# Second product of MLP 1 by Strassen's seven products, and spatial weights prepared in MLP 2

## The chip, the cores and the metric

One core of a Trainium2 chip runs the whole program. The metric is the device time of one execution in microseconds; lower is better. Everything is float32 on the host. TensorE works on fp32r copies: each operand is split in a high part and a low part (value minus high part), and a product is three matmuls, high x high, low x high, high x low.

## The reference

```python
# attention, 4 batches x 8 heads x 576 x 64, with rotary q and k; then, per batch of 576 x 512:
xn = (x - mu) / np.sqrt(var + 1e-06) * g_ln          # MLP 1
x = x + np.maximum(xn @ w_ch1, 0.0) @ w_ch2          # 512 -> 2048 -> 512
h = gelu(x @ w_in)                                   # MLP 2, 512 -> 1024
u, v = (h[..., :512], h[..., 512:])
v_n = (v - mu) / np.sqrt(var + 1e-06) * g_ln
v_s = np.einsum('ts,bsd->btd', w_sg, v_n) + b_sg[None, :, None]
x = x + (u * v_s) @ w_out
```

## The kernel before

The program has three stages: attention over 16 pairs of heads, written as software-pipelined rounds; MLP 1; MLP 2. Each engine has its own instruction stream, in an order written out by hand, and waits on semaphores. Data of all stages stays in SBUF.

MLP 1 works in five blocks of rows. Block 0 and blocks 2 to 4 hold the first 512 rows of one batch each (`block_tiles` = 4 tiles of 128 rows); block 1, the tails block, holds the last 64 rows of the four batches in 2 tiles. All 2048 hidden features are 16 tiles (NF). In a block TensorE alternates `hidden(n, f)` (L1624, matmul at L1637: 12 matmuls of 512 columns, 256 in the tails block, one PSUM bank of two) with `project(n, f - 1)` (L1642, matmul at L1652: 4 row tiles x 3 matmuls of 512 columns into the four banks of `acc_ps`, which gather over all 16 f). Between them ScalarE's relu writes the high part of `hid` (L946) and DVE the low part (L1268). At the end of a block DVE adds the four banks to Y (L1288).

The next block's input is made beside this: DVE's statistics at f = 4, GpSimd's `inverse_std` (L759, the power -0.5), DVE's `normalise` at f = 8 (L1175); then TensorE transposes xhat in four groups (`transpose_x`, L1576), two before the last-but-one `project` and two before the last, into the two banks of `xT_ps`; ScalarE (L933) and DVE (L1183) read each bank out as high and low part of xT. Block 0's x is transposed during attention.

Weights of MLP 1: SP loads slices of W1 and W2 for one f at a time into two raw slots (L644, L645); in block 0 ScalarE writes the high parts (L938, L939) and DVE the low parts (L1242, L1244), two f ahead; GpSimd did the first two f during the last rounds of attention. They stay in SBUF for all blocks. `hidden(0, 0)` stands in the last round of attention; behind the rounds come `transpose_o_tails` (L1661, the attention output of the tails, 16 transposes), DVE's merging of them (L1259), `hidden(0, 1)`, `project(0, 0)` and so on.

In the last block w_in and w_out are loaded and split between the steps (L961, L966, L1297, L1302); at f = 10 to 14 TensorE also transposes the spatial weights w_sg in five groups (`transpose_spatial`, L1700) into `xT_ps`, ScalarE (L975) and DVE (L1309) split them into wsT; and at the end Y of batch 0 is transposed (L1710, L1717) and split (L994, L1318).

MLP 2 goes batch by batch: `v_tiles` (L1737, 12 matmuls of 512 columns per row tile), `u_chunks` (L1757), the transposes of the next batch, `spatial` (L1775), the next batch's `v_tiles`, `outputs` (L1789). Each v tile goes through gelu on ScalarE (L1011) and, in DVE's queue, `v_stats` (L1335, L1337, L1339), GpSimd's power (L812) and `v_normal` (L1344, L1350, L1352); DVE takes the statistics of tile t ahead of the normalising of tile t - 1.

## Time and profile before

| | |
|---|---|
| median of 3 runs | 941.87 us (940.79 to 942.12) |
| the profiled execution's own time | 940.78 us |
| its span | 939.0 us |
| granted TensorE clock | 1.0 of full speed (2.4 GHz) over the span |
| attention | up to about 313 us |
| MLP 1 | about 313 to 720 us |
| MLP 2 | about 720 us to the end |

The span is what the profiler's records cover; the remaining 1.8 us of the execution lie around it. Engines are named PE (TensorE matmul), PEld (its weight loads), DVE, ACT (ScalarE), POOL (GpSimd), SPq (the queue that issues DMAs). Matmuls overlap, so that the duration of one is longer than the distance to the next.

### The profile page before, as it was taken

How to read it: one execution, taken by the hardware profiler on the slowest of the kernel's cores; microseconds unless marked ns; L12 is line 12 of the kernel's file. 1: busy time of each engine (PE TensorE's matmuls, PEld its weight loads, DVE VectorE, ACT ScalarE, POOL GpSimd, SP SyncE). 2: the span in 40 equal slices, each digit the busy share in tenths (PEclk: the TensorE clock that was granted, in tenths of full speed). 3: DMA queues.
4: the chain of work that ended last, by engine and by line, in shares of the span. 5: the costliest groups of instructions: out<-in, count | busy, mean ns of one | idle time of the engine just before them, and what ended most of it. 6: DMA issues, size and time to landing. Idle time of an engine off the chain costs nothing.

```text
span 939.0 us, 15729 instructions
## 1 busy us (share of the span) xinstructions
PE 914.4 (97%) x5577; PEld 820.3 (87%) x5577; DVE 510.9 (54%) x903; ACT 400.0 (43%) x857; POOL 269.2 (29%) x249
## 2 busy tenths in 40 slices
PE   4899999999999999999999999999999999999998
PEld 3899999999989888898888888888888999989897
DVE  5899999999998644232222322132235663663623
ACT  4899999999988332211111111121123221302110
POOL 4989989989863000000000000000000110010100
PEclk9999999999999999999999999999999999999999
DMA  6243243233222332100000000003100001010011
GB/s 177 65 103 93 66 102 91 64 102 92 67 56 71 105 100 90 68 1 1 1 1 0 1 0 0 0 1 114 45 1 1 1 1 45 2 45 13 1 45 57
DMA packets 44966, 44.24 MB, mean 47 GB/s; under 512 B 14128, under 2 KB 34864, under 8 KB 44784
## 3 DMA queue, kind: packets, MB, share of 16 engines
q1 hardware_dynamic: 44480, 43.21, 16.5%
q8 instruction: 35, 0.57, 0.2%
q10 hardware_dynamic: 432, 0.30, 0.1%
q14 instruction: 19, 0.16, 0.1%
HBM read 28.81 MB, written 4.72 MB: 36 GB/s over the span
## 4 chain that ended last, share of the span: by engine, by line
PE 91%; DVE 4%; issue 1%; POOL 1%; ACT 1%; DMA 0%; SPq 0%; POOLq 0%; ACTq 0%; DVEq 0%
PE hid_ps L1637 21%; PE acc_ps L1652 21%; PE ring_ps L1545 8%; PE wide_ps L1775 6%; PE scores_ps L1481 6%; PE wide_ps L1757 5%; PE ring_ps L1492 5%; PE bank_ps L1789 5%; PE bank_ps L1737 5%; PE scores_ps L1474 2%; PE ring_ps L1428 2%; DVE nmax L1105 1%; PE ring_ps L1558 1%; PE ring_ps L1503 1%; DVE prob_lo L1114 1%
## 5 line engine op out<-in xcount | busy, mean ns | idle before, releaser
L1652 PE MATMUL acc_ps<-W2s,hid 128*128 128x512 f32 x864 | 210.6, 391 | 0.1
L1637 PE MATMUL hid_ps<-xT,W1s 128*128 128x512 f32 (+1 forms) x960 | 210.4, 369 | 0.3 <-DVE xT L1183 0.3
L1637 PEld LDWEIGHTS hid_ps<-xT,W1s 128*128 128x128 f32 x960 | 168.6, 188 | 31.9 <-issue 0.7
L1652 PEld LDWEIGHTS acc_ps<-W2s,hid 128*128 128x128 f32 x864 | 160.5, 188 | 33.1 <-DVE hid L1268 0.8
L1268 DVE SCALAR_TENSOR_TENSOR hid<-hid_ps,hid 128x512 fp32r<-128x512 f32 (+1 forms) x80 | 51.0, 638 | 253.1 <-ACT hid L946 253.0
L946 ACT ACTIVATE hid<-hid_ps 128x512 fp32r<-128x512 f32 (+1 forms) x80 | 44.4, 555 | 304.3 <-PE hid_ps L1637 304.3
L1105 DVE TENSOR_REDUCE nmax<-scores_ps 128x1 f32<-128x576 f32 x144 | 106.8, 752 | 14.1 <-PE scores_ps L1481 10.3
L812 POOL TENSOR_TENSOR rstd<-ve,power 128x1 f32<-128x1 f32 x18 | 14.6, 814 | 306.1 <-DVE ve L1339 306.1
L855 ACT ACTIVATE E<-scores_ps,nmax 128x576 f32<-128x576 f32 x128 | 95.7, 749 | 11.5 <-DVE nmax L1105 10.8
L1114 DVE TENSOR_TENSOR prob_lo<-ring_ps,prob_hi 128x512 fp32r<-128x512 f32 x144 | 95.4, 681 | 2.1 <-ACT prob_hi L869 1.7
L869 ACT ACTIVATE prob_hi<-ring_ps 128x512 fp32r<-128x512 f32 x144 | 85.6, 613 | 2.3 <-PE ring_ps L1492 0.9
L1481 PE MATMUL scores_ps<-stack 128*128 128x288 f32 x256 | 80.1, 328 | 0.9 <-ACT E L855 0.9
L1492 PE MATMUL ring_ps<-ident,E 128*128 128x128 f32 x512 | 76.7, 276 | 1.5 <-DVE prob_lo L1114 1.4
L759 POOL TENSOR_TENSOR rstd<-ve,power 128x4 f32<-128x4 f32 (+1 forms) x5 | 4.8, 954 | 251.7 <-DVE ve L1168 251.7
L1545 PE MATMUL ring_ps<-prob_hi,v_split 128*128 128x288 f32 x256 | 76.2, 316 | 0.2 <-DVE prob_lo L1114 0.2
L1481 PE MATMUL scores_ps<-swapped_k,stack 128*128 128x288 f32 x256 | 72.2, 297 | 0.0
L1545 PE MATMUL ring_ps<-prob_lo,v_split 128*128 128x288 f32 x256 | 70.8, 295 | 0.0
L1492 PEld LDWEIGHTS ring_ps<-ident,E 128*128 128x128 f32 x512 | 58.7, 140 | 3.6 <-issue 1.8
L1775 PE MATMUL wide_ps<-wsT,v_hat 128*128 128x288 f32 x448 | 60.3, 295 | 0.0
L1775 PEld LDWEIGHTS wide_ps<-wsT,v_hat 128*128 128x128 f32 x448 | 59.6, 188 | 0.0
L1757 PEld LDWEIGHTS wide_ps<-yT,winS 128*128 128x128 f32 x384 | 51.3, 188 | 0.3
L1757 PE MATMUL wide_ps<-yT,winS 128*128 128x288 f32 x384 | 51.5, 294 | 0.0
(142 smaller groups left out, 1441.6 us busy)
## 6 DMA issues: line engine op xcount, KB each, us to landing
swapped_k<-stack SPq DMA_DIRECT2D x64, 144.0 KB, 2.4
w_raw<-in_w SPq DMA_DIRECT2D x32, 256.0 KB, 3.0
qk_raw<-in_k SPq DMA_DIRECT2D x16, 256.0 KB, 2.7
v_raw<-in_v SPq DMA_DIRECT2D x16, 256.0 KB, 2.8
qk_raw<-in_q SPq DMA_DIRECT2D x15, 256.0 KB, 2.8
out<-out_sb SPq DMA_DIRECT2D x14, 256.0 KB, 2.2
w_raw<-in_win SPq DMA_DIRECT2D x4, 512.0 KB, 4.2
rotary<-rotary_table SPq DMA_DIRECT2D x2, 576.0 KB, 4.3
```

What stands on the lines that cost most here:

```text
L855: nc.scalar.activation(dst, src, ACT.Exp, bias=nmax[:, s:s + 1], accum_out=rowsum[:, p.odd, s:s + 1]).then_inc(expd, 1)
L869: nc.scalar.activation(dst, src, ACT.Copy).then_inc(prob_hi_s, 1)
L1105: nc.vector.tensor_reduce(nmax[:, s:s + 1], scored(p, s), axis=AX.X if s == NT else AX.XY, op=ALU.max, negate=True).then_inc(maxed, 1)
L1114: read_out(nc.vector.tensor_tensor(dst, src, hi.bitcast(f32), ALU.subtract), job, h)
L1268: nc.vector.scalar_tensor_tensor(out=hid[:, f % 2, 1, 0:cols], in0=hid_ps[:, f % 2, 0:cols], scalar=0.0, in1=hid[:, f % 2, 0, 0:cols].bitc ...
L1481: mm = nc.tensor.matmul(ps[:, half, 0:HALF], queries, keys, start=(m == 0), stop=(m == 1))
L1492: mm = nc.tensor.transpose(bank(f"G{t}", h)[:, P * c:P * c + P], E[:, t, at + P * c:at + P * c + P], ident[:, :])
L1545: mm = nc.tensor.matmul(bank(job, h)[:, 0:HALF], values, moving, start=(c == 0 and n == 0), stop=(c == NT and n == 1))
L1637: mm = nc.tensor.matmul(hid_ps[:, f % 2, 0:cols], W1s[:, slot1(f), w, c, :], xT[:, x, c, 0:cols], start=first, stop=(c == DC - 1 and x == 1))
L1652: mm = nc.tensor.matmul(acc_ps[:, t, :], hid[:, f % 2, x, P * t:P * t + P], W2s[:, slot2(f), w, :], start=(f == 0 and x == 0 and w == 0), ...
L1757: mm = nc.tensor.matmul(wide_ps[j % 2][:, half, 0:HALF], winS[:, c, w, P * j:P * j + P], yT[:, a, c, HALF * half:HALF * (half + 1)], start ...
L1775: mm = nc.tensor.matmul(wide_ps[j % 2][:, half, 0:HALF], v_hat[:, a, c, P * j:P * j + P], wsT[:, w, c, HALF * half:HALF * (half + 1)], sta ...
```

## The change

The second product of MLP 1 goes by pairs of hidden tiles (g, eight of them) and pairs of row tiles. The 2x2 blocks are: hidden tiles 2g and 2g + 1 against even and odd row tiles on the left, W2's two row tiles against the two halves of its 512 columns on the right. Seven products of (128 rows x 128) by (128 x 256), by the variant of Strassen's method with 4 + 4 sums ahead, gather in seven PSUM banks `seven_ps` over all g. The left factors (`lefts`) come from ScalarE's relu and high parts and DVE's four sums and five low parts; the right factors (`rights`), made anew for every pair in every block, from GpSimd's four sums of W2 and four low parts, ScalarE's five high parts and one low part on DVE. `lefts`, `rights`, `w2_sums`, `hid`, `hid_sums` have one buffer each. At the end of a block eight `fold` steps on DVE, two copies on ScalarE and four additions on GpSimd bring the seven banks into Y. W2 is no longer split as a whole; it is kept raw, loaded for two f at a time.

With seven banks taken, one bank (`fc1_ps`) is left for `hidden` and for the four groups of x transposes, which now stand one by one between products. Half of `transpose_o_tails` stands behind `hidden(0, 1)`. The spatial weights are transposed and split inside `v_tiles(0)` and use the banks of `wide_ps`, which `u_chunks(0)` needs next. The blocks, which were in part a loop, are written out. The core of the diff, with the outer indentation taken off (in the order SP, GpSimd, ScalarE, DVE, TensorE):

```diff
-hid = sbuf(m1, "hid", [P, 2, 2, NT * P], f32r)
+hid = sbuf(m1, "hid", [P, 2, NT * P])
+hid_sums = sbuf(m1, "hid_sums", [P, 4, 2 * P])
 W1s = sbuf(m1, "W1s", [P, NF, 2, DC, P], f32r)
-W2s = sbuf(m1, "W2s", [P, NF, 2, DM], f32r)
+w2_rest = sbuf(m1, "w2_rest", [P, NF - 2, DM])
+lefts = sbuf(m1, "lefts", [P, SEVEN, 2, 2 * P], f32r)
+folds = sbuf(m1, "folds", [P, 2, 4 * P])
+rights = sbuf(m1, "rights", [P, SEVEN, 2, 2 * P], f32r)
+w2_sums = sbuf(m1, "w2_sums", [P, 4, 2 * P])
...
-acc_ps = psum(m1_ps, "acc_ps", [P, NT, 512])
-hid_ps = psum(m1_ps, "hid_ps", [P, 2, 512])
-xT_ps = psum(m1_ps, "xT_ps", [P, 2, 512])
+seven_ps = {n: psum(m1_ps, f"seven_ps{n}", [P, 512]) for n in range(3, SEVEN)}
+fc1_ps = psum(m1_ps, "fc1_ps", [P, 512])
+seven_ps.update({n: psum(m1_ps, f"seven_ps{n}", [P, 512]) for n in range(3)})
...
+SPATIAL = ((), (0, 1), (2,), (3,), (4,))
...
+def y_bank(b, c):
+    return bank_ps[0 if b == 0 else c]
...
+LEFT_PARTS = (1, 2, 3, 3, 4, 5, 5)
+FOLDS = 8
+FREE_FOLDS = (3, 2, 4, 5, 6, 7, 8)
...
-        sp.wait_ge(w_lo, max(2 * (f - 1), 4))
+        sp.wait_ge(w_lo, f - 1)
         load_weights(f)
-    sp.wait_ge(w_lo, 2 * NF)
-    for c in range(2):
-        sp.dma_start(pass_raw[c], win_v[:, c, :]).then_inc(raw_in[c], 16)
-    sp.wait_ge(fc2, (NBLK - 1) * NF + SG1)
-    sp.dma_start(wsg_raw[:, 0:NT, :], wsg[0:NT * P, :].rearrange("(p t) s -> p t s", t=NT)).then_inc(wsg_in, 16)
...
+        if f == 2:
+            wait_filled(sp, pair(PAIRS - 1), ("PV0", 0), ("PV1", 0), ("PV0", 1), ("PV1", 1))
+        if f % 2 == 0:
+            sp.dma_start(w2_rest[:, f - 2:f, :], w2_v[:, f:f + 2, :]).then_inc(w2_in[f // 2 - 1], 16)
+    def wait_rights(count):
+        sp.wait_ge(right_lo, 4 * count)
+        sp.wait_ge(right_lo_sums, count)
+    sp.wait_ge(w_lo, NF)
+    sp.dma_start(pass_raw[0], win_v[:, 0, :]).then_inc(raw_in[0], 16)
+    wait_rights((NBLK - 1) * NG + 1)
+    sp.dma_start(pass_raw[1], win_v[:, 1, :]).then_inc(raw_in[1], 16)
     for c in range(2, DC):
         sp.wait_ge(mw_lo, c - 1)
         sp.dma_start(pass_raw[c % 2], win_v[:, c, :]).then_inc(raw_in[c % 2], 16)
     for c in range(0, DC, 2):
         sp.wait_ge(mw_lo, DC - 1 + c // 2)
...
+    wait_rights((NBLK - 1) * NG + 5)
...
+    def weight_sums(n, g):
+        at = n * NG + g
+        if at == 0:
+            pool.wait_ge(scores, PAIRS * NQK)
+            pool.wait_ge(w_in[1], 32)
+        if n == 0 and g > 0:
+            pool.wait_ge(w2_in[g - 1], 16)
+        if at > 0:
+            pool.wait_ge(right_lo_sums, at)
+            pool.wait_ge(right_lo, 4 * at)
+        sums = [w2_sums[:, m, :] for m in range(4)]
+        w11, w12, w21, w22 = [w2_block(g, f, half) for f in range(2) for half in range(2)]
+        nc.gpsimd.tensor_tensor(sums[T3], w22, w12, ALU.subtract).then_inc(w2_summed, 1)
+        nc.gpsimd.tensor_tensor(sums[T1], w12, w11, ALU.subtract).then_inc(w2_summed, 1)
+        pool.wait_ge(w2_summed, 4 * at + 2)
+        nc.gpsimd.tensor_tensor(sums[T2], w22, sums[T1], ALU.subtract).then_inc(w2_summed, 1)
+        pool.wait_ge(w2_summed, 4 * at + 3)
+        nc.gpsimd.tensor_tensor(sums[T4], sums[T2], w21, ALU.subtract).then_inc(w2_summed, 1)
+    def right_low(n, g, k):
+        pool.wait_ge(right_hi, 5 * (n * NG + g) + {0: 1, 1: 2, 2: 3, 6: 5}[k])
+        src = {0: w2_block(g, 0, 0), 1: w2_sums[:, T3, :], 2: w2_block(g, 1, 0), 6: w2_block(g, 1, 1)}[k]
+        nc.gpsimd.tensor_tensor(rights[:, k, 1, :], src, rights[:, k, 0, :].bitcast(f32), ALU.subtract).then_inc(right_lo, 1)
+    def add_to_y(n, odd, half, m, wait):
+        pool.wait_ge(folded, FOLDS * n + wait)
+        y = y_block(n, odd, half)
+        nc.gpsimd.tensor_tensor(y, y, fold_view(n, folds[:, m, :]), ALU.add).then_inc(y1_done, 1)
+    weight_sums(0, 0)
+    for k in (0, 1, 2, 6):
+        right_low(0, 0, k)
+    for n in range(NBLK):
+        for g in range(NG):
+            ahead = after(n, g)
+            if ahead[0] < NBLK:
+                weight_sums(*ahead)
+                for k in range(3):
+                    right_low(*ahead, k)
+            if g == NG - 1:
+                add_to_y(n, 1, 1, 0, 2)
+            if ahead[0] < NBLK:
+                right_low(*ahead, 6)
+            if g == 3 and not is_last(n):
+                inverse_std(n + 1)
+        pool.wait_ge(y1_done, 4 * n + 1)
+        add_to_y(n, 1, 1, 1, 6)
+        add_to_y(n, 1, 0, 0, 7)
+        add_to_y(n, 0, 1, 1, 8)
...
-    def weights_high(f):
-        act.wait_ge(w_in[f % 2], 32 * (f // 2 + 1))
+    def w1_high(f):
+        act.wait_ge(w_in[f % 2], 16 * (f // 2 + 2))
         nc.scalar.activation(W1s[:, slot1(f), 0, :, :], w1_raw[:, f % 2, :, :], ACT.Copy).then_inc(w_hi, 1)
-        nc.scalar.activation(W2s[:, slot2(f), 0, :], w2_raw[:, f % 2, :], ACT.Copy).then_inc(w_hi, 1)
...
+    def relu(n, g, f):
+        at = n * NG + g
         cols = P * block_tiles(n)
+        act.wait_ge(fc1, 2 * at + f + 1)
+        if at > 0:
+            if f == 0:
+                act.wait_ge(hid_summed, 4 * (at - 1) + 3)
+            else:
+                act.wait_ge(left_lo, 5 * (at - 1) + 3)
+        nc.scalar.activation(hid[:, f, 0:cols], fc1_ps[:, 0:cols], ACT.Relu).then_inc(hid_relu, 1)
...
+    def left_high(n, g, part):
+        at = n * NG + g
+        wait_product(n, g, (0, 1, 3, 4, 6)[part])
...
+        nc.scalar.activation(dst, src, ACT.Copy).then_inc(left_hi, 1)
...
+    def right_high(n, g, part):
+        at = n * NG + g
+        wait_product(n, g, (0, 1, 2, 5, 6)[part])
...
+        if part == 1:
+            act.wait_ge(w2_summed, 4 * at + 1)
+        if part == 3:
+            act.wait_ge(w2_summed, 4 * at + 4)
+            dst, src = rights[:, 3:6, 0, :], w2_sums[:, T4:T2 + 1, :]
+        else:
+            dst = rights[:, (0, 1, 2, 0, 6)[part], 0, :]
+            src = {0: w2_block(g, 0, 0), 1: w2_sums[:, T3, :], 2: w2_block(g, 1, 0), 4: w2_block(g, 1, 1)}[part]
+        nc.scalar.activation(dst, src, ACT.Copy).then_inc(right_hi, 1)
...
+    def copy_fold(n, m):
+        k = (0, 4)[m]
+        act.wait_ge(fc2, SEVEN * (n * NG + NG - 1) + k + 1)
+        if n > 0:
+            act.wait_ge(y1_done, 4 * n)
+        nc.scalar.activation(folds[:, m, 0:2 * P * block_pairs(n)], seven(n, k), ACT.Copy).then_inc(fold_copied, 1)
...
+    def factors(n, g):
+        first, last = n > 0 and g == 0, g == NG - 1
+        if first:
+            copy_fold(n - 1, 0)
+        if n == 0 and g == 0:
+            w1_high(2)
+            for part in range(5):
+                right_high(0, 0, part)
+        relu(n, g, 0)
+        if n == 0 and 0 < g and 2 * g + 2 < NF:
+            w1_high(2 * g + 2)
+        left_high(n, g, 0)
+        right_high_beside(n, g, 0)
+        if last:
+            relu(n, g, 1)
+        left_high(n, g, 1)
+        right_high_beside(n, g, 1)
+        if last:
+            next_high(n, 0)
+        right_high_beside(n, g, 2)
+        if first:
+            copy_fold(n - 1, 1)
+        if not last:
+            relu(n, g, 1)
+        if n == 0 and 2 * g + 3 < NF:
+            w1_high(2 * g + 3)
+        left_high(n, g, 2)
+        if last:
+            next_high(n, 1)
+        left_high(n, g, 3)
+        right_high_beside(n, g, 3)
+        if last:
+            next_high(n, 2)
+        left_high(n, g, 4)
+        right_high_beside(n, g, 4)
+        if last:
+            next_high(n, 3)
+            next_high(n, 4)
...
+    def spatial_high(c):
+        if c == 0:
+            act.wait_ge(y1_done, 4 * NBLK)
+        act.wait_ge(wsT_ps, c + 1)
...
+    def hid_sum(n, g, m):
+        at = n * NG + g
+        if m == S3:
+            if at > 0:
+                dve.wait_ge(left_lo, 5 * at)
+            dve.wait_ge(hid_relu, 2 * at + 1)
+            a, b, op = hid_rows(n, 0, 0), hid_rows(n, 1, 0), ALU.subtract
+        elif m == S1:
+            dve.wait_ge(hid_relu, 2 * at + 2)
+            a, b, op = hid_rows(n, 1, 0), hid_rows(n, 1, 1), ALU.add
+        elif m == S2:
+            dve.wait_ge(hid_summed, 4 * at + 2)
+            a, b, op = sum_rows(n, S1), hid_rows(n, 0, 0), ALU.subtract
+        else:
+            dve.wait_ge(hid_summed, 4 * at + 3)
+            a, b, op = hid_rows(n, 0, 1), sum_rows(n, S2), ALU.subtract
+        nc.vector.tensor_tensor(sum_rows(n, m), a, b, op).then_inc(hid_summed, 1)
+    def left_low(n, g, part):
+        dve.wait_ge(left_hi, 5 * (n * NG + g) + part + 1)
...
+        nc.vector.tensor_tensor(dst, src, high.bitcast(f32), ALU.subtract).then_inc(left_lo, 1)
...
+    def fold(n, step):
+        k = (0, 1, 0, 2, 3, 5, 5, 6)[step]
+        dve.wait_ge(fc2, SEVEN * (n * NG + NG - 1) + k + 1)
+        if step in (0, 1, 5):
+            dve.wait_ge(fold_copied, 2 * n + 1 + step // 5)
...
+    def factors(n, g):
+        first, last = n > 0 and g == 0, g == NG - 1
+        if first:
+            for step in range(4):
+                fold(n - 1, step)
+        if n == 0 and g == 0:
+            w1_low(2)
+            merge_tails((0, 1))
+        hid_sum(n, g, S3)
+        left_low(n, g, 0)
+        if n == 0 and 0 < g and 2 * g + 2 < NF:
+            w1_low(2 * g + 2)
+        if not last:
+            left_low(n, g, 1)
+        if first:
+            fold(n - 1, 4)
+        if n == 0 and g == 0:
+            w1_low(3)
+            merge_tails((2, 3))
+            right_low_sums(0, 0)
+        hid_sum(n, g, S1)
+        hid_sum(n, g, S2)
+        hid_sum(n, g, S4)
+        if last:
+            left_low(n, g, 1)
+            next_low(n, 0)
+        left_low(n, g, 2)
+        if n == 0 and 0 < g and 2 * g + 3 < NF:
+            w1_low(2 * g + 3)
+        if last:
+            next_low(n, 1)
+        left_low(n, g, 3)
+        if n > 0 or g > 0:
+            right_low_sums(n, g)
+        if first:
+            fold(n - 1, 5)
+            fold(n - 1, 6)
+        if last:
+            next_low(n, 2)
+        left_low(n, g, 4)
+        if first:
+            fold(n - 1, 7)
+        if last:
+            next_low(n, 3)
+            next_low(n, 4)
...
             if t > 0:
                 v_normal(jobs_tv(b) + t - 1, b, t - 1)
+            if b == 0 and t < count:
+                for c in SPATIAL[t]:
+                    spatial_low(c)
...
+            elif c == 0:
+                pe.wait_ge(hid_relu, n * NF)
             else:
-                if isinstance(n, int) and n == 1 and c < 2:
-                    wait_bank_done((1, 2)[c])
-                head_wait(pe, xT_lo, n, DC, c - 1)
+                pe.wait_ge(xT_lo, n * DC + c)
...
-    def project(n, f):
-        pe.wait_ge(hid_lo, n * NF + f + 1)
-        if f == 0:
-            head_wait(pe, y1_done, n, 1, 0)
-            if isinstance(n, int) and n == 0:
-                pe.wait_ge(tails_merged, B)
-                pe.wait_ge(w_lo, 4)
-        for t in range(block_tiles(n)):
+    def product(n, g, k):
+        at = n * NG + g
+        pe.wait_ge(left_lo, 5 * at + LEFT_PARTS[k])
+        if 3 <= k < 6:
+            pe.wait_ge(right_lo_sums, at + 1)
+        else:
+            pe.wait_ge(right_lo, 4 * at + min(k + 1, 4))
+        if g == 0 and n > 0:
+            pe.wait_ge(folded, FOLDS * (n - 1) + FREE_FOLDS[k])
+        elif g == 0 and k < 3:
+            wait_bank_done(k)
+        elif g == 0:
+            pe.wait_ge(tails_merged, B)
+        for a in range(block_pairs(n)):
             for x, w in ((0, 0), (1, 0), (0, 1)):
-                mm = nc.tensor.matmul(acc_ps[:, t, :], hid[:, f % 2, x, P * t:P * t + P], W2s[:, slot2(f), w, :],
-                                      start=(f == 0 and x == 0 and w == 0), stop=(f == NF - 1 and w == 1))
+                mm = nc.tensor.matmul(seven_ps[k][:, 2 * P * a:2 * P * (a + 1)], lefts[:, k, x, P * a:P * (a + 1)],
+                                      rights[:, k, w, :], start=(g == 0 and a == 0 and x == 0 and w == 0),
+                                      stop=(g == NG - 1 and a == block_pairs(n) - 1 and w == 1))
         mm.then_inc(fc2, 1)
...
+    def products(n, g):
+        steps = [("fc1", 0), 0, 1, 2, ("fc1", 1), 3, 4, 5, 6]
+        if g == NG - 2:
+            steps = [("fc1", 0), 0, ("fc1", 1), 1, ("x", 0), 2, 3, ("x", 1), 4, 5, ("x", 2), 6]
+        elif is_last(n) and g == NG - 1:
+            steps = [0, ("x", 3), 1, 2, ("tails", 0), 3, 4, 5, 6]
+        elif g == NG - 1:
+            steps = [0, ("x", 3), 1, 2, ("fc1", 0), 3, 4, ("fc1", 1), 5, 6]
+        m, h = after(n, g)
...
     rounds(pe, body, (-2, 1))
-    transpose_o_tails()
-    def mlp1_block(n):
...
-            if f == NF - 1 and not is_last(n):
-                transpose_x(n + 1, range(2))
...
-            project(n, f - 1)
-            if is_last(n) and SG2 < f <= SG2 + NTT:
-                transpose_spatial(f - SG2 - 1)
-        if not is_last(n):
-            transpose_x(n + 1, range(2, DC))
-        else:
...
+    transpose_o_tails((0, 1))
+    hidden(0, 1)
+    transpose_o_tails((2, 3))
...
     def transpose_spatial(c):
         if c == 0:
             pe.wait_ge(wsg_in, 32)
-        else:
-            pe.wait_ge(wsT_lo, c)
+            pe.wait_ge(folded, FOLDS * NBLK)
+        if c >= 2:
+            pe.wait_ge(wsT_lo, c - 1)
         rows = P if c < NT else TAIL
-        dst = xT_ps[:, :, :].rearrange("p a n -> p (a n)")
+        dst = wide_ps[c % 2][:, :, :].rearrange("p a n -> p (a n)")
...
+            if b == 0:
+                for c in SPATIAL[t]:
+                    transpose_spatial(c)
...
             elif b > 0:
                 pe.wait_ge(sg_bias, DC * b - 1 + j)
-            elif j == 0:
-                pe.wait_ge(y1_done, NBLK)
+            else:
+                pe.wait_ge(wsT_lo, NTT - j)
```

## Rows read from the trace of the kernel before

**Rows 1.** The page: busy time by engine, and the chain that ended last.

```profile
PE 914.4 (97%) x5577; PEld 820.3 (87%) x5577; DVE 510.9 (54%) x903; ACT 400.0 (43%) x857; POOL 269.2 (29%) x249
...
PE 91%; DVE 4%; issue 1%; POOL 1%; ACT 1%; DMA 0%; SPq 0%; POOLq 0%; ACTq 0%; DVEq 0%
```

**Rows 2.** Groups by shape, PE: count | busy us, mean ns | idle before.

```profile
L1652 PE MATMUL acc_ps<-W2s,hid 128*128 128x512 f32 x864 | 210.6, 391 | 0.1
...
L1637 PE MATMUL hid_ps<-xT,W1s 128*128 128x256 f32 x192 | 25.4, 283 | 0.0
```

**Rows 3.** PE's timeline (start us, us) in block 3 and in the tails block.

```profile
634.26 2.88 PE L1637 MATMUL hid_ps<-xT,W1s 128*128 128x512 f32 x12
636.98 2.88 PE L1652 MATMUL acc_ps<-W2s,hid 128*128 128x512 f32 x12
...
404.98 1.59 PE L1637 MATMUL hid_ps<-xT,W1s 128*128 128x256 f32 x12
406.41 1.55 PE L1652 MATMUL acc_ps<-W2s,hid 128*128 128x512 f32 x6
407.80 1.59 PE L1637 MATMUL hid_ps<-xT,W1s 128*128 128x256 f32 x12
```

**Rows 4.** Groups by shape, POOL, with two inputs in SBUF.

```profile
L712 POOL TENSOR_TENSOR cross<-qk_raw,rotary 128x288 f32<-128x288 f32 x60 | 47.5, 818 | 0.0
...
L768 POOL TENSOR_TENSOR W1s<-w_raw,W1s 128x512 fp32r<-128x512 f32 x2 | 2.6, 1302 | 0.2
```

**Rows 5.** Timeline 12 to 14.2 us, DVE and POOL; and one line's min/median/max.

```profile
12.19 0.41 DVE L1062 TENSOR_TENSOR qk_split<-rot,qk_split 128x256 fp32r<-128x256 f32 x1
...
12.78 1.40 POOL L697 TENSOR_TENSOR rot<-qk_raw,rotary 128x576 f32<-128x576 f32 x1 [11.79 <-DVE qk_split L1062]
12.84 1.61 DVE L1062 TENSOR_TENSOR qk_split<-rot,qk_split 128x256 fp32r<-128x256 f32 x1
...
14.13 0.98 POOL L712 TENSOR_TENSOR cross<-qk_raw,rotary 128x288 f32<-128x288 f32 x1
...
L712 POOL TENSOR_TENSOR cross<-qk_raw,rotary x4: 792/806/982, 14.1 to 18.0; 128x288 f32<-128x288 f32 x4
```

**Rows 6.** PE's timeline at the end of block 0: x transposes for the tails block.

```profile
394.04 0.60 PE L1576 MATMUL xT_ps<-ident,xhat 128*128 128x128 f32 x4
394.39 3.00 PE L1652 MATMUL acc_ps<-W2s,hid 128*128 128x512 f32 x12
397.24 0.60 PE L1576 MATMUL xT_ps<-ident,xhat 128*128 128x128 f32 x4
```

**Rows 7.** Groups by shape, ACT and DVE.

```profile
L933 ACT ACTIVATE xT<-xT_ps,g1c 128x512 fp32r<-128x512 f32 x12 | 7.6, 686 | 5.7 <-PE xT_ps L1576 5.6
...
L1183 DVE SCALAR_TENSOR_TENSOR xT<-xT_ps,g1c,xT 128x512 fp32r<-128x512 f32 x12 | 8.4, 746 | 5.5 <-ACT xT L933 5.5
...
L1242 DVE TENSOR_TENSOR W1s<-w_raw,W1s 128x512 fp32r<-128x512 f32 x14 | 9.7, 691 | 4.2 <-ACT W2s L939 4.2
...
L1309 DVE TENSOR_TENSOR wsT<-xT_ps,wsT 128x576 fp32r<-128x576 f32 x4 | 3.0, 758 | 8.4 <-ACT wsT L975 8.4
```

**Rows 8.** Timeline at the start of MLP 1, all engines.

```profile
310.44 0.58 SPq L644 DMA_DIRECT2D w_raw<-in_w  x1
...
314.13 0.63 ACT L938 ACTIVATE W1s<-w_raw 128x512 fp32r<-128x512 f32 x1 [0.82 <-DMA w_raw<-in_w]
...
314.62 3.02 PE L1637 MATMUL hid_ps<-xT,W1s 128*128 128x512 f32 x12
```

**Rows 9.** Timelines: spatial transposes in block 4; start of MLP 2.

```profile
683.22 0.89 PE L1700 MATMUL xT_ps<-ident,wsg_raw 128*128 128x128 f32 x5
...
733.81 12.88 PE L1757 MATMUL wide_ps<-yT,winS 128*128 128x288 f32 x96
...
729.20 0.69 DVE L1335 BATCH_NORM_STATS2 stats<-v_act 128x6 f32<-128x512 f32 x1
...
731.25 0.69 DVE L1352 TENSOR_TENSOR v_hat<-v_act,v_hat 128x512 fp32r<-128x512 f32 x1
```

425 lines of the change are left out of this document (257 added, 168 removed).

## The prediction

> **What bounds the kernel now.** I read the page's busy shares and the chain that ended last first: TensorE is busy 97% of the span and carries 91% of the chain [rows 1]. Then the groups by shape: the second product is 864 matmuls of 512 columns [rows 2]. Then TensorE's timeline for the pitch, which a busy sum hides since matmuls overlap: in a block of four tiles 12 matmuls start every 2.72 us, 227 ns each; in the tails block 12 of 256 columns start every 1.43 us (119 ns), 6 of 512 every 1.39 us [rows 3]. Nothing waits there. So TensorE's time is the kernel's, column or wait alike. Last I read what one DVE, ScalarE or GpSimd instruction takes, as the change gives these three work in every step.
>
> **Part 1, matmuls.** Per pair of hidden tiles a full block goes from 24 matmuls of 512 columns (5.44 us) to 7x2x3 = 42 of 256. At 119 ns [rows 3] that is 5.01 us: 0.43 saved, 32 times, 13.9 us. In the tails block 12 of 512 (2.78) become 21 of 256 (2.50): 8x0.28 = 2.2. Together **-16.1 us**. (Columns fall by 1/8, but each matmul carries some 13 ns besides them, and their number rises from 864 to 1512.)
>
> **Part 2, GpSimd, and its port with DVE.** Each pair of hidden tiles gives GpSimd eight instructions of 256 columns (four sums of W2, four low parts), in every block anew. Its rows give 818 ns for 288 columns and 1302 for 512 [rows 4], so about 0.75 for 256, and back to back they follow some 50 ns closer (14.13 against an end at 14.18 [rows 5]): 0.70. Two of the sums wait for the one before, 0.15 each: 5.9 us per pair. A full block's pair takes TensorE 5.44+5.01 = 10.45 us, so there it is hidden. The tails block's takes 2.86+2.50 = 5.4: **GpSimd becomes the bound**, since w2_sums and rights have one buffer and weight_sums waits for all low parts of the pair before.
> DVE's new instructions (four sums, five low parts of the left, one of the right) have both inputs in SBUF. The trace has such a one against GpSimd: the subtraction of 256 columns takes 0.41 us alone, but 1.61 where it starts 0.06 us after a GpSimd instruction that ends at 14.18, and the next GpSimd instruction takes 0.98 where its like take 0.81 [rows 5]. They don't run together. So DVE takes from GpSimd 0.17 for 256 columns. A tails pair has 2176 such columns: 1.4 us in proportion, 2.3 at the 1.08 ns per column that 0.41 for 256 and 0.69 for 512 [rows 7] make; I take 1.9. Period 5.9+1.9 = 7.8.
> From the Trainium skill, SBUF — State Buffer, section "Who interferes with whom": the port pair is an exclusive lock held for the whole instruction, where a DVE instruction has two SBUF inputs and GpSimd reads SBUF. By that to the letter the whole durations add up, and the period would be about 9 us, the total 8 us more than below; the row shows GpSimd losing less, and I keep 7.8.
> The tails block, from its predecessor's last product: fc1 and products of the first pair 5.5 us, but GpSimd has first three additions into Y of 512 columns (1.3 each [rows 4], the first after DVE's sixth fold at about 2.2) till 6.0, then four sums and a low part, 3.7 and 0.7 for DVE's holds, so that product 0 of the second pair can start at 10.4 and the pair ends at 15.4. Four periods of 7.8 to the sixth; 1.0 for inverse_std in GpSimd's queue; then two pairs with x transposes. There each step must pass transposes 0.60, ScalarE 0.69, DVE 0.75 and handshakes 0.1, 2.15 us to the next step [rows 6, 7], before the single bank fc1_ps is free, while TensorE has only 1.2 us of other work (0.35 transposes, 0.13 for the switch, two products of 0.36): with the 512-column fc1 of the next block 20.5 us for the two pairs. 15.4+31.2+1.0+20.5 = 68.1 against 47.4 of pure TensorE work (14x1.43, 2x2.72, 8x2.50, transposes 1.9): **+20.7**. Bounds: +5 (GpSimd hidden, only the x chain waits) and +35 (period 9.3).
>
> **Part 3, x transposes between full blocks.** Before, eight transposes stood together in two banks, and four cost 0.35, with 0.13 for the switch to matmuls and back (2.85 to the next start instead of 2.72) [rows 6]. Now four at a time share one bank with fc1. The same chain of 2.15 is met by 1.92 of cover (0.35+0.13+2x0.72): 0.2 short per step. DVE's queue has three sums and a low part ahead of the first low part of x (+0.3), the right's low part of 768 columns ahead of the third (+0.3), and fc1 waits for relu twice (+0.3); two more switches (+0.2): 1.7, and 1.0 for GpSimd in DVE's way. Two such boundaries 5.4; into the tails block 2.9; y's transposes at the end 2.8: **+11.1**. Bounds +4 and +16. At a full block's start the folds (8x0.69 on DVE [rows 7], beside 3584 columns of its own, 3.9, in the 10.4 us of a pair) and additions are met by nearly a whole pair of slack: **+1.0** for both, bounds 0 and 4.
>
> **Part 4, start.** ScalarE's order puts W1's third slice and five high parts of the right ahead of relu(0,0). The slice is issued at 310.44 and was cast at 314.13 (then also behind W2's) [rows 8]; without W2 I take 313.4. 0.5+1.8 us of copies, relu 0.6: hidden(0,1), which before started at 314.62 behind all tail transposes, now waits till 316.4 where TensorE is ready at 313.8. Product 2 then waits 0.7 for DVE (W1 low, merges, right low, three sums). Less the wait of 0.5 that goes: **+2.8**, bounds 0 and 5. SP's queue keeps its order there; W2's 0.5 MB loads are a pair ahead of use. W2's splits (14 each on ScalarE and DVE) go; they lay beside TensorE and give nothing back.
>
> **Part 5, spatial weights.** 25 transposes move from the last block into v_tiles(0); TensorE's cost is the same. u_chunks(0) now waits for the fifth low part, behind gelu, statistics and the normalising of a tile in DVE's queue: gelu with its handshake 0.8, statistics to low part 729.20 to 731.94 = 2.74 [rows 9], wsT 0.76 [rows 7], handshakes 0.1, less the 0.89 of the transposes beside it [rows 9]: **+3.5**, bounds 2.5 and 5. Spatial products of batch 0 have the u products, 12.9 us [rows 9], before them. SP's loads of w_in, w_out and w_s now wait for rights or low parts of the last block, each at least a pair of 10.4 us ahead of its use, and its queue has nothing else then: 0; if one came late, every later load behind it would too. ScalarE: 12 instructions with 4608 columns, 6.2 us per full pair at the 0.69 for 512 of [rows 7], in 10.4: hidden. Unrolled blocks: only instruction fetch, 0.
>
> **Sum:** -16.1+20.7+11.1+1.0+2.8+3.5 = +23.0. The profiled execution has 940.78 (span 939.0), 1.1 below the median of 941.87: 963.8, on the median's scale 964.9. Some of these waits will overlap with one another, so I say **960**.
>
> **Rivals.**
> A, the cover holds: GpSimd and DVE run far enough ahead, transposes hide; only start and end cost. 941.9-16.1+6.3 = 932. For it: they idle most of this stage today. Against: single buffers keep them from running ahead, and 5.9 > 5.4. Chance 0.12. It decides if GpSimd's 256 columns take 0.6 or less and DVE is not in its way.
> B, the port costs nothing, as today in MLP 1, where GpSimd idles: period 5.9 (4x1.9 less, and about 2 more where the block starts and ends), no 1.0 at each of four boundaries: 963.8-13.6 = 950. Chance 0.18. Against it: rows 5.
> C, the lock also fills the full blocks: GpSimd 5.9, DVE's 3584 two-input columns 3.9 and in block 0 its W1 parts, 10 and more, with waits for each other's ends: 1 us over on 32 pairs, 995. Chance 0.09. Decides where a full pair's period passes 10.45.
> D, Strassen saves nothing: if 256 columns cost 132 ns, as their busy sum over count says (25.4/192) [rows 2], 42 take 5.55, more than 5.44; 1512x0.013 = 20 us more than my case, 980. The timeline (12 in 1.43) speaks against. Chance 0.03.
> E, waits just use up the saving: 942. Chance 0.05.
> My own case, 950 to 975: 0.53.
>
> **Numbers.** The range leaves out A and C (0.21) and holds the bounds of the big terms in part: 938 to 985. What this kernel's measurement can tell from no change is about 0.2%, 1.9 us. Faster 0.13 (A and a little of B's lower side), same 0.05, slower 0.82.
>
> **What would show it.** (1) Product rows of 256 columns pitched 0.119. (2) In the tails block a period near 7.8, GpSimd busy nearly throughout, TensorE waiting for the right's low part. (3) GpSimd rows of 256 columns longer than 0.75 on average and DVE rows of 256 with two SBUF inputs up to 1.1 long. (4) TensorE waits of 0.2 to 1 before each x transpose group. (5) One wait of 3 to 4 us before the first u product; one of 2 to 3 before hidden(0,1). I am wrong if GpSimd's rows stay at 0.74 and the tails block keeps TensorE's pace, or if full pairs exceed 10.45 in the middle of a block.

## The result, and the profile after

The changed kernel takes 984.4 us (median of 4 runs, 982.35 to 985.15) against 942.0 for the kernel before on the same chip: ratio 1.045, 95% interval 1.043 to 1.047. The forecast was 960, slower; the direction is right and 984.4 lies in the range of 938 to 985, at its edge. The rise is 42 us where the working gave 23, so most of this section and the next is about the other 20. The profiled execution, the longest of the four, has a span of 983.4. Below, fc1 is the first product of MLP 1 (`hidden`, twelve matmuls), and x transposes are the four groups that prepare the next block's input.

The page of the kernel after, busy time and chain, against [rows 1]:

```profile
PE 928.7 (94%) x6225; PEld 857.4 (87%) x6225; DVE 755.3 (77%) x1231; ACT 566.4 (58%) x1253; POOL 570.0 (58%) x585
...
PE 79%; DVE 12%; ACT 3%; issue 2%; POOL 2%; DMA 1%; SPq 0%; ACTq 0%; DVEq 0%; POOLq 0%
```

DVE now carries 12% of the chain, GpSimd only 2%. That is the first sign against the prediction, which had named GpSimd. The next lines are windows of MLP 1, cut where the first fc1 of a block starts; they hold block 0, the tails block, block 2 and block 3. Their columns are: window, us, then busy us and count of TensorE, its weight loads, DVE, ScalarE, GpSimd; granted clock; DMA share and GB/s.

```profile
310.99:407.21 96.22, 88.80 (x535) 78.68 (x533) 77.13 (x115) 53.21 (x116) 57.59 (x67) 0.96 0.28 83
...
407.21:481.14 73.93, 57.26 (x391) 54.39 (x389) 63.78 (x107) 38.24 (x102) 57.86 (x71) 0.86 0.00 1
481.14:570.91 89.77, 88.06 (x533) 78.20 (x533) 66.26 (x107) 48.39 (x102) 58.14 (x69) 0.98 0.00 1
570.91:659.81 88.90, 87.19 (x544) 78.18 (x544) 72.58 (x107) 48.69 (x102) 61.46 (x70) 1.00 0.00 1
```

Block 3 takes 88.9, as a full block did before (88.86 between the same places): what the products save there is given back at the block's end, no more and no less. The tails block takes 73.9, with TensorE busy 57 of them and DVE 64; TensorE's work in that window, some 390 matmuls at the pitch of 0.12, is about 46 (an estimate). Now TensorE's timeline, against [rows 3, 6, 8]: the start of MLP 1, a full pair, and the tails block from its fourth pair.

```profile
318.13 4.42 PE L1986 MATMUL fc_ps<-xT,W1s 128*128 128x512 f32 x12 [2.93 <-ACT hid L1066]
...
329.98 0.98 PE L2007 MATMUL seven_ps<-rights,lefts 128*128 128x256 f32 x6 [2.23 <-DVE lefts L1529]
330.80 4.51 PE L1986 MATMUL fc_ps<-xT,W1s 128*128 128x512 f32 x12
335.15 3.03 PE L2007 MATMUL seven_ps<-rights,lefts 128*128 128x256 f32 x24
338.02 2.91 PE L1986 MATMUL fc_ps<-xT,W1s 128*128 128x512 f32 x12
...
440.01 2.40 PE L1986 MATMUL fc_ps<-xT,W1s 128*128 128x256 f32 x12 [3.31 <-ACT hid L1066]
...
457.45 2.70 PE L1986 MATMUL fc_ps<-xT,W1s 128*128 128x256 f32 x12 [4.59 <-ACT hid L1066]
```

24 matmuls of 256 columns, 335.15 to 338.02, are pitched 0.12, as forecast, and a full pair lasts 10.51 (335.15 to 345.66). But twelve fc1 matmuls of 512 columns last 4.42 and 4.51 behind a wait and 2.91 elsewhere. The granted clock (the last column but two) is below 1.00 there, so the engine ran in part at 1.2 GHz:

```profile
315.00:320.00 5.00, 2.07 (x7) 1.51 (x6) 3.88 (x9) 3.79 (x9) 3.25 (x4) 0.78 0.83 267
330.00:335.00 5.00, 5.00 (x18) 4.10 (x19) 3.52 (x6) 2.10 (x6) 3.02 (x4) 0.66 0.10 30
```

And TensorE waits in the tails block for ScalarE's relu. The relu stands behind a left part in ScalarE's queue, and these parts wait for DVE's sums of hid, 15.6 us in 422 to 474:

```profile
L1088 ACT ACTIVATE lefts<-hid_sums 128x128 fp32r<-128x128 f32 x12 | 3.7, 310 | 15.8 <-DVE hid_sums L1517 15.6 <-PE seven_ps L2007 0.2
```

The groups by shape of DVE, then of GpSimd, against [rows 4, 5, 7]:

```profile
L1517 DVE TENSOR_TENSOR hid_sums<-hid 128x256 f32<-128x256 f32 x64 | 47.4, 741 | 45.7 <-ACT hid L1066 45.5
...
L1529 DVE TENSOR_TENSOR lefts<-hid,lefts 128x256 fp32r<-128x256 f32 x40 | 32.8, 819 | 0.1
...
L1554 DVE TENSOR_TENSOR Y<-seven_ps,Y 128x512 f32<-128x512 f32 x20 | 13.2, 680 | 0.1
```

```profile
L898 POOL TENSOR_TENSOR rights<-w_rest,rights 128x256 fp32r<-128x256 f32 x105 | 97.7, 933 | 74.9 <-ACT rights L1107 74.9
```

DVE's 256 columns with two inputs in SBUF take 0.74 and 0.82 in these groups (0.62 to 0.64 in the other three) where 0.41 is the time alone, while a 512-column one with an input in PSUM stays at 0.68. In MLP 2 the forecast wait of 3.5 stands as 3.60, and the 96 u products behind it take 14.28 instead of 12.9:

```profile
775.70 14.28 PE L2130 MATMUL wide_ps<-yT,winS 128*128 128x288 f32 x96 [3.60 <-DVE wsT L1650]
```

### The profile page after: what moved, and what is told of

Its sections match the earlier page's. It is cut to its first block, busy times and chain, and to the rows that moved or that the text cites. A ratio compares the mean times of both kernels' runs of the same rounds, so it can differ in the third digit from the quotient of the medians.

```text
span 983.4 us, 18631 instructions
## 1 busy us (share of the span) xinstructions
PE 928.7 (94%) x6225; PEld 857.4 (87%) x6225; DVE 755.3 (77%) x1231; ACT 566.4 (58%) x1253; POOL 570.0 (58%) x585
## 4 chain that ended last, share of the span: by engine, by line
PE 79%; DVE 12%; ACT 3%; issue 2%; POOL 2%; DMA 1%; SPq 0%; ACTq 0%; DVEq 0%; POOLq 0%
PE fc_ps L1986 18%; PE seven_ps L2007 13%; PE ring_ps L1893 7%; PE scores_ps L1829 6%; PE wide_ps L2151 6%; PE wide_ps L2130 5%; PE ring_ps L1840 5%; PE bank_ps L2165 5%; PE bank_ps L2107 4%; DVE hid_sums L1517 3%; PE scores_ps L1822 2%; PE ring_ps L1776 2%; DVE lefts L1529 1%; DVE xT L1421 1%; ACT rights L1107 1%
## 5 line engine op out<-in xcount | busy, mean ns | idle before, releaser
L1986 PE MATMUL fc_ps<-xT,W1s 128*128 128x512 f32 (+1 forms) x960 | 221.5, 382 | 15.3 <-ACT hid L1066 14.6
L1986 PEld LDWEIGHTS fc_ps<-xT,W1s 128*128 128x128 f32 x960 | 170.3, 197 | 46.6 <-ACT hid L1066 13.9
L2007 PE MATMUL seven_ps<-rights,lefts 128*128 128x256 f32 x1512 | 204.2, 288 | 2.8 <-DVE lefts L1529 2.2
L2007 PEld LDWEIGHTS seven_ps<-rights,lefts 128*128 128x128 f32 x1512 | 196.6, 195 | 8.9 <-DVE lefts L1529 2.9
L898 POOL TENSOR_TENSOR rights<-w_rest,rights 128x256 fp32r<-128x256 f32 x105 | 97.7, 933 | 74.9 <-ACT rights L1107 74.9
L1088 ACT ACTIVATE lefts<-hid_sums 128x256 fp32r<-128x256 f32 (+2 forms) x120 | 54.8, 457 | 78.8 <-DVE hid_sums L1517 71.1
L1517 DVE TENSOR_TENSOR hid_sums<-hid 128x256 f32<-128x256 f32 (+1 forms) x80 | 56.6, 707 | 50.9 <-ACT hid L1066 50.4
L1066 ACT ACTIVATE hid<-fc_ps 128x512 f32<-128x512 f32 (+1 forms) x80 | 44.0, 550 | 82.4 <-PE fc_ps L1986 82.3
L1529 DVE TENSOR_TENSOR lefts<-hid_sums,lefts 128x256 fp32r<-128x256 f32 (+2 forms) x120 | 86.0, 717 | 2.2 <-ACT lefts L1088 2.2
L1529 DVE TENSOR_TENSOR lefts<-hid,lefts 128x256 fp32r<-128x256 f32 (+1 forms) x80 | 62.8, 785 | 0.1
```

The source lines that it names most:

```text
L898: nc.gpsimd.tensor_tensor(rights[:, k, 1, :], src, rights[:, k, 0, :].bitcast(f32), ALU.subtract).then_inc(right_lo, 1)
L1517: nc.vector.tensor_tensor(sum_rows(n, m), a, b, op).then_inc(hid_summed, 1)
L1529: nc.vector.tensor_tensor(dst, src, high.bitcast(f32), ALU.subtract).then_inc(left_lo, 1)
L1986: mm = nc.tensor.matmul(fc1_ps[:, 0:cols], W1s[:, slot1(f), w, c, :], xT[:, x, c, 0:cols], start=first, stop=(c == DC - 1 and x == 1))
L2007: mm = nc.tensor.matmul(seven_ps[k][:, 2 * P * a:2 * P * (a + 1)], lefts[:, k, x, P * a:P * (a + 1)], rights[:, k, w, :], start=(g == 0 an ...
```

## The experiments

e1 to e4 and e8 are single executions. The changed kernel's own four lie 2.8 us apart, so these five are read from their blocks first and from their totals second.

**Whose work fills the tails block (e1, e2).** Theory 1: DVE and GpSimd block each other there, DVE's bursts add waits, and the lost clock adds time. Two kernels leave one side's work out, all but 8 columns of each instruction, without a change in order or waits.

```diff
# e1: GpSimd's sums and low parts, e2: DVE's sums and low parts of the tails block
+cols = slice(0, 8 if n == 1 else 2 * P)
-nc.gpsimd.tensor_tensor(rights[:, k, 1, :], src, ...)
+nc.gpsimd.tensor_tensor(rights[:, k, 1, cols], src[:, cols], ...)
```

> Leaves out: in the tails block GpSimd's eight instructions of a pair (four sums of W2, four low parts) work on 8 of their 256 columns; order and semaphores stay. The tails block takes 74.5 us (without the fc1 of its successor above a tails fc1) where pure TensorE work is 47.4. Theory 1 (the shared port lengthens DVE's instructions, DVE's bursts stop the hidden sums, and each TensorE idle stretch costs clock as well): DVE's rows of 128 and 256 columns in that block fall to 0.29 and 0.42, the block to 60 to 66, the kernel to 970 to 976. Rival, GpSimd's amount of work bounds the period: the block to 50 to 55, the kernel to 960 to 965. Rival, ScalarE and the handshakes bound it: under 4 us less, 980 or more.

> Leaves out: in the tails block DVE's four sums of hid, five low parts of the left and the low part of the right work on 8 columns of each row group; GpSimd's work, statistics, normalising and folds stay. Theory 1: GpSimd's 256-column rows in that block fall from 0.80 to 0.90 towards 0.74; the waits behind the statistics, the normalising and the folds stay (2 to 4 us each, three of them), as does the low clock behind them; the block falls from 74.5 to 62 to 68, the kernel to 971 to 978. Rival, GpSimd bounds it by itself: the block falls by under 4. Rival, DVE's small work bounds it: the block to 50 to 55, the kernel to 960 to 965.

Without GpSimd's columns: 968.97 us, the tails block 58.1. Its window, and DVE's groups in its middle (421.4 to 458):

```profile
407.91:465.97 58.06, 50.57 (x391) 48.76 (x389) 42.68 (x107) 37.36 (x102) 22.67 (x69) 0.95 0.01 1
```

```profile
L1519 DVE TENSOR_TENSOR hid_sums<-hid 128x128 f32<-128x128 f32 x13 | 3.9, 302 | 7.8 <-ACT hid L1068 7.6
...
L1531 DVE TENSOR_TENSOR lefts<-hid,lefts 128x256 fp32r<-128x256 f32 x6 | 2.5, 419 | 0.0
L1395 DVE BATCH_NORM_STATS2 stats<-Y 128x6 f32<-128x512 f32 x4 | 2.5, 673 | 0.0
...
L1415 DVE TENSOR_SCALAR xhat<-Y,mv,rstd 128x512 f32<-128x512 f32 x4 | 1.9, 546 | 0.9 <-POOL rstd L837 0.9
```

The same groups of the changed kernel (422 to 474):

```profile
L1517 DVE TENSOR_TENSOR hid_sums<-hid 128x128 f32<-128x128 f32 x13 | 7.8, 600 | 4.5 <-ACT hid L1066 4.3
L1529 DVE TENSOR_TENSOR lefts<-hid,lefts 128x256 fp32r<-128x256 f32 x7 | 5.6, 802 | 0.0
...
L1413 DVE TENSOR_SCALAR xhat<-Y,mv,rstd 128x512 f32<-128x512 f32 x4 | 3.5, 944 | 0.6 <-POOL rstd L837 0.6
L1393 DVE BATCH_NORM_STATS2 stats<-Y 128x6 f32<-128x512 f32 x4 | 2.5, 674 | 0.0
```

DVE did the same instructions in 42.7 instead of 63.8 us: 21 us of DVE's "busy" time in that block was waiting for GpSimd. Without DVE's columns the kernel takes 973.56, the block 64.6, and GpSimd's low parts go from 828 to 747 ns. Its timeline shows how GpSimd holds DVE:

```profile
434.70 0.74 POOL L898 TENSOR_TENSOR rights<-w_sums,rights 128x256 fp32r<-128x256 f32 x1
434.87 0.60 DVE L1518 TENSOR_TENSOR hid_sums<-hid_sums,hid 128x8 f32<-128x8 f32 x1
435.40 0.75 POOL L898 TENSOR_TENSOR rights<-w_rest,rights 128x256 fp32r<-128x256 f32 x1
435.50 0.67 DVE L1518 TENSOR_TENSOR hid_sums<-hid,hid_sums 128x8 f32<-128x8 f32 x1
436.10 0.16 DVE L1534 TENSOR_TENSOR lefts<-hid,lefts 128x16 fp32r<-128x16 f32 x1
```

A DVE instruction of 8 columns that needs 0.16 lasts 0.60 and 0.67, until GpSimd's ends. Four pairs in the middle of the tails block, in the changed kernel, in e1 and in e2 (columns as above):

```profile
422.08:457.45 35.37, 27.04 (x180) 26.04 (x180) 31.35 (x55) 17.60 (x48) 29.19 (x37) 0.86 0.00 1
421.38:446.85 25.47, 23.59 (x180) 23.19 (x181) 18.75 (x55) 16.95 (x48) 9.02 (x34) 0.93 0.01 2
420.86:450.39 29.53, 24.03 (x180) 22.18 (x181) 20.43 (x55) 17.18 (x48) 26.66 (x37) 1.00 0.01 1
```

The block without GpSimd's columns came out 2 us below what theory 1 expected, the other within it; the rival "ScalarE and handshakes" is out, since the block falls by 16; "GpSimd by itself bounds it" is out, since taking DVE's columns away gives 9.4; so is "DVE's small work bounds it", which wanted 50 to 55. Neither side alone accounts for the block.

**Bursts or sums (e3).** The same work with DVE's statistics one tile per pair, and the normalising in two halves.

```diff
-elif g == 2:
-    for t in range(block_tiles(n + 1)):
-        tile_statistics(n + 1, t)
+elif g < 4:
+    t = g - 4 + block_tiles(n + 1)
+    if t >= 0:
+        tile_statistics(n + 1, t)
...
-elif g == 4:
-    normalise(n + 1)
+elif g < 6:
+    normalise(n + 1, range(half * (g - 4), half * (g - 3)))
```

> The same work in another order: in every block DVE takes the statistics of one tile per pair of hidden tiles (pairs 0 to 3) and normalises half of the tiles behind pair 4 and half behind pair 5, instead of all at once behind pair 2 and pair 4. Theory 1: the waits of 3.3 and 4.6 us before fc1 in the tails block shrink to under 1 us each, and the 2.4 to 2.5 us that the fc1 behind them takes goes back to 1.6; the block loses 6 to 9 us, the kernel comes to 975 to 979. Rival, the block is bound by GpSimd's eight instructions: they fill the gap, the block loses under 2. Other stages stay within 1 us.

978.4 us, within the expected numbers and for the wrong reason. The block:

```profile
403.40:475.69 72.29, 56.46 (x391) 52.02 (x389) 63.06 (x107) 37.90 (x102) 58.36 (x71) 0.91 0.00 1
```

It lost 1.6, the rival's figure: the waits of 3.31 and 4.59 before fc1 became several of 0.4 to 2.9, and DVE is busy as long as before (63.1). So the bursts are worth 1.6 at most, and what is left fits the sum of DVE's held-up instructions. About 3 us came at the start, which the edit hardly touches: behind nearly the same two waits the clock stayed up this time. TensorE's timeline there:

```profile
317.21 2.99 PE L1989 MATMUL fc_ps<-xT,W1s 128*128 128x512 f32 x12 [2.71 <-ACT hid L1066]
...
327.63 0.98 PE L2010 MATMUL seven_ps<-rights,lefts 128*128 128x256 f32 x6 [2.23 <-DVE lefts L1529]
```

**The clock (e8).** In the three long waits of the tails block TensorE is kept at work by matmuls that nothing reads.

```diff
+for _ in range({(1, 1): 22, (1, 3): 24, (1, 5): 34}.get((n, g), 0)):
+    nc.tensor.matmul(seven_ps[0][:, 2 * P:4 * P], W1s[:, slot1(0), 0, 0, :], xT[:, 0, 0, 0:2 * P], start=False, stop=False)
```

> Only the clock: in the changed kernel's tails block, in the three places where TensorE waits 2.95, 3.31 and 4.59 us before fc1, it issues 22, 24 and 34 matmuls of 256 columns (0.119 each) that add into columns which nothing reads. The waits shrink to about 0.4 and the matmuls behind them run at full clock: 12 in 1.6 instead of 2.4 to 2.9. If TensorE's lost clock lies on the path, the block loses 3 to 5 us; if DVE and GpSimd set the period there and TensorE waits for them anyway, it loses under 1.

The window of the tails block:

```profile
407.43:481.05 73.62, 63.48 (x470) 58.86 (x468) 64.56 (x107) 38.01 (x102) 57.76 (x70) 0.95 0.00 1
```

The fc1 behind the waits go back from 2.4 and 2.7 to 1.70, the clock from 0.86 to 0.95, and the block takes 73.62 instead of 73.93: behind those three waits the lost clock is free, since DVE sets the pace. 984.16 us in all. Theory 1 falls in this part. The slow stretch at the block's end, with its x transposes, stayed as it was; this run says nothing about it.

**Start and first u products (e4).**

```diff
+relu(n, g, 0)
 if n == 0 and g == 0:
     w1_high(2)
     for part in range(5):
         right_high(0, 0, part)
-relu(n, g, 0)
...
+for _ in range(14):        # ahead of the wait for the spatial weights
+    nc.tensor.matmul(bank_ps[1][:, :], yT[:, 0, 0, 0:P], winS[:, 0, 0, DM:2 * DM], start=True, stop=True)
```

> Two edits in stages far apart. At the start ScalarE's relu(0,0,0) stands ahead of W1's third slice and the five high parts of the right. Before the first u product TensorE, instead of idling for the fifth low part of the spatial weights, issues 14 matmuls of 512 columns (0.227 each, 3.2 us) into a bank that nothing reads. Theory 1: the wait of 2.93 us before hidden(0,1) falls under 0.5, its 12 matmuls take 2.9 instead of 4.42, though the wait for DVE before product 2 grows by up to 1.5; in sum 2 to 4 us. The u products start when they did, and the 96 of batch 0 take 12.9 instead of 14.28, 1.4 less. Kernel 979 to 981. Rival, the clock has nothing to do with the idle stretch before: the u products stay at 14.3, and the fc1 at 4.4.

979.33 us. Both effects are there: block 0 takes 92.6 instead of 96.2 (the wait is 2.2 shorter and the fc1 behind it 1.45), and the u products (384 in the program) need 51.7 instead of 53.0 busy us, with TensorE at work instead of waiting before them. TensorE's timeline at the start, then the group of the u products:

```profile
314.55 3.02 PE L1986 MATMUL fc_ps<-xT,W1s 128*128 128x512 f32 x12
...
319.17 2.97 PE L1986 MATMUL fc_ps<-xT,W1s 128*128 128x512 f32 x12 [0.73 <-ACT hid L1066]
...
325.84 0.98 PE L2007 MATMUL seven_ps<-rights,lefts 128*128 128x256 f32 x6 [2.27 <-DVE lefts L1529]
326.65 4.50 PE L1986 MATMUL fc_ps<-xT,W1s 128*128 128x512 f32 x12
```

```profile
L2134 PE MATMUL wide_ps<-yT,winS 128*128 128x288 f32 x384 | 51.7, 295 | 0.1
```

Here, where TensorE itself is the bound, the clock costs: 1.5 per fc1 of 512 columns behind a wait, 1.3 at the u products.

**Plain products in the tails block (e5).** Slots 0, 1, 2 and 6 of the right hold W2's four blocks, slots 0 to 3 of the left hid's; no sums there.

```diff
+PLAIN = (((0, 0, 0, 0),), ((0, 1, 0, 1), (1, 0, 1, 0)), ((1, 1, 1, 1),),
+         ((2, 2, 0, 0),), ((3, 2, 1, 0),), ((2, 6, 0, 1), (3, 6, 1, 1)), ())
...
+for left, right, tile, half in PLAIN[k]:
+    for x, w in ((0, 0), (1, 0), (0, 1)):
+        nc.tensor.matmul(seven_ps[tile][:, 2 * P * half:2 * P * (half + 1)], lefts[:, left, x, 0:P], rights[:, right, w, :], ...)
```

> In the tails block the second product goes by its four plain blocks (24 matmuls of 256 columns per pair instead of 21), in two banks; no sums of hid or of W2 there, and per pair GpSimd has four low parts (3.0 us alone), DVE 512 columns of left low parts instead of 2176. Full blocks keep Strassen. Between the first fc1 of the tails block and that of its successor the changed kernel has 73.9 us, the one with GpSimd's work shrunk 58.1. Theory 1, DVE and GpSimd holding each other up there: TensorE's work is 8 x 5.73 + 1.9, with the x transposes' waits about 53; I expect 51 to 57, the kernel 963 to 969. Rival, the single bank fc1_ps, relu and the handshakes hold the period: over 62, the kernel over 972.

975.0 us, ratio 1.0345 (1.032 to 1.037), 9.4 less than the changed kernel: less than expected, and over the rival's 972. The block takes 61.0, between the theory's 57 and the rival's 62. No wait stands in it until the x transposes, which then wait 1.07, 1.81, 2.01 and 1.30 on their single bank, so the rival's bank holds the block's end and not its period. Block 2 grew from 89.8 to 94.3. The cause of that stands in the timelines of the combined kernel below: the edit had put the tails' fold, which waits for the last product, ahead of the next block's first sum of hid.

**x transposes (e6, e9).** Two ways of spreading them: only DVE's and ScalarE's order, then TensorE's as well.

```diff
# e6
+if last:
+    left_low(n, g, 1)
+    next_low(n, 0)
 hid_sum(n, g, S1)
...
# e9, TensorE
-steps = [("fc1", 0), 0, ("fc1", 1), 1, ("x", 0), 2, 3, ("x", 1), 4, 5, ("x", 2), 6]
+steps = [("fc1", 0), 0, ("fc1", 1), 1, ("x", 0), 2, 3, 4, ("x", 1), 5, 6]
...
-steps = [0, ("x", 3), 1, 2, ("fc1", 0), 3, 4, ("fc1", 1), 5, 6]
+steps = [0, ("x", 2), 1, 2, ("x", 3), 3, 4, ("fc1", 0), 5, 6, ("fc1", 1)]
```

> In the last pair of each block DVE reads out the first group of x (or y) transposes ahead of its three sums of hid, and ScalarE ahead of the right's second high part. Theory 1: the wait of 0.87 before the second group of x transposes in each full block (2.9 in the tails block, 0.8 for y) goes or falls under 0.3, unless the second product's left parts come late for it; 0.5 to 0.7 less at each full boundary, 1 to 2.5 less at the tails block's end; kernel 979 to 982.5. Rival, the chain transposes, ScalarE, DVE itself is what lasts, not DVE's queue: 983.5 or more.

> The changed kernel, with the x (and y) transposes of a block's end spread further: the four groups stand behind products 1 and 4 of the last-but-one pair and behind products 0 and 2 of the last, the first fc1 of the next block behind product 4, and ScalarE and DVE read each out as soon as their order allows. By the chain of 2.15 us per step (transposes, ScalarE, DVE, handshakes) against three products and a switch, 2.65, the waits of 0.87, 0.23 and 0.40 at each full boundary fall to under 0.4 in sum, 1 us or more per boundary; the tails block's end gains 1 to 3; kernel 977 to 981. Rival, as in the run before that only moved DVE's order, one wait takes the place of another: over 982.

e6 gives 981.85 (ratio 1.0428, 1.041 to 1.0445), but in its profile the gain lies in block 0 (93.65), not where it was expected. Most of it, 1.6 us, is the clock again, behind the same wait of 2.23 as in the changed kernel:

```profile
329.98 2.90 PE L1986 MATMUL fc_ps<-xT,W1s 128*128 128x512 f32 x12
```

Block 3 takes 88.98. The first wait went from 0.88 to 0.24 and the second from 0.23 to 1.16. e9 gives 984.9 (1.0449, 1.043 to 1.047): two waits of 0.48 and 0.62 remain, one of 0.69 before the next fc1 is new, block 3 takes 89.44. The mechanism of both rivals came out, one wait in another's place; e6's total lies in theory 1's range all the same, by the clock in block 0. With one bank for fc1 and x a full boundary kept its cost in the three orders tried.

**Everything together (e7, e10).** Start order (in DVE's first step the left's third low part ahead of W1's slice too), spread statistics, plain tails block, x read out early, spatial groups one v tile earlier (`SPATIAL = ((), (0, 1), (2, 3), (4,), ())`). The second version moves the plain fold, gives block 2's x transposes four of the banks that are free in the plain tails block, takes e9's steps, and in the first step puts W1's slice, two merges and the right's low part behind the sums.

```diff
# e10 against e7
+if n == 2:
+    return seven_ps[2 + c][:, :]     # xT_bank
...
+hid_sum(n, g, S3)
+left_low(n, g, 0)
 if first and n == 2:
     for step in range(2):
         fold(n - 1, step)
-hid_sum(n, g, S3)
-left_low(n, g, 0)
```

> Together: relu first at the start, and in DVE's first step the left's third low part ahead of W1's slice, the merges and the sums; statistics and normalising spread; plain products in the tails block; x read out early; the spatial weights' groups one v tile earlier (none behind the last). By stage, if the savings add up: start 6 to 8 less than the changed kernel, tails block 18 to 22, the three other boundaries 2, waits and slow u products in MLP 2 about 5: 984.4 - 34 = 950, range 945 to 955. If the causes overlap (one wait behind another), 955 to 962. The kernel before has 942: Strassen in four full blocks saves 13.9, of which the boundaries' four single-bank transposes take 2.9 each, so at best it comes level.

> The combined kernel with three repairs: the x transposes as in the run beside it, but those behind the plain tails block in four banks that are free there; the two plain folds behind the first hidden sum and low part of the next block; in the first step W1's slice, merges and the right's low part behind the sums. Expected by stage: tails block 59.4 to 49 or 51, block 2 93.85 to 89 or less (wait of 3.31 and the 4.60 that the fc1 behind it takes both go), the other boundaries 1 each, the start 1. 964 - 10 - 5 - 3 = 946, range 940 to 952. Level with the kernel before (941.7) only if all waits go: the pairs save 0.37 each (10.51 against 10.88), 32 times 12 us, and the boundaries, the start and MLP 2 give back at least 2 per block.

e7: 964.2 us, ratio 1.0244 (1.023 to 1.026), outside the range of 945 to 955 and above the 955 to 962 given for causes that overlap. Its timeline at the start of block 2 names the missing part:

```profile
467.53 1.29 DVE L1581 TENSOR_TENSOR Yt<-seven_ps,Yt 128x512 f32<-128x512 f32 x2 [8.60 <-PE seven_ps L2056]
468.73 0.41 DVE L1550 TENSOR_TENSOR hid_sums<-hid 128x256 f32<-128x256 f32 x1
...
470.80 4.60 PE L2036 MATMUL fc_ps<-xT,W1s 128*128 128x512 f32 x12 [3.31 <-ACT hid L1084]
```

DVE waits 8.6 us at the fold, the sum and thus relu stand behind it, TensorE waits 3.31 and then runs slowly. e10 takes 952.0 us, ratio 1.011 (1.009 to 1.013), at the upper end of its range: the tails block 52.6 instead of e7's 59.4 (49 to 51 expected), block 2 88.8 instead of 93.9 (89 or less expected). Its edits came together, so no run parts the four banks from e9's steps. The tails block and the two blocks behind it:

```profile
398.85:451.47 52.62, 50.80 (x408) 48.91 (x406) 26.30 (x50) 26.18 (x77) 31.56 (x40) 1.00 0.01 1
...
451.47:540.25 88.78, 86.78 (x538) 77.43 (x539) 62.88 (x101) 48.32 (x101) 56.80 (x67) 1.00 0.00 1
540.25:629.73 89.48, 87.50 (x545) 78.20 (x545) 71.23 (x107) 48.71 (x102) 62.92 (x69) 1.00 0.00 1
```

Of the changed kernel's 42 us, 32 are gone, and 21 of these are the tails block's. The full blocks with Strassen still take what they took before, so no version tried here beats the kernel before.

## Why the prediction was right in direction and short in size

By its own parts; "measured" is from windows of the two profiled executions cut at like places. The rise was 44.4 between the spans where the working gave 23.0, and the largest part of what is missing, 9.3 us, lies in part 2.

- **Part 1** held: the pitch is 0.12 and a full pair lasts 10.51 against the forecast 10.45. Rivals D (Strassen saves nothing) and E (no change) are out.
- **Part 3** held for full boundaries: blocks 2 and 3 changed by -0.9 and 0.0 us, where the terms give about -0.5 each. That the saving is just used up there is the quiet half of the result.
- **Part 5**: 3.60 against 3.5. Missed: the clock behind that wait, +1.4.
- **Part 4**, start: the wait before hidden(0,1) is 2.93, forecast 2.6. The wait of product 2 was put at 0.7 and is 2.23: W1's slice, both merges, the right's low part of 0.96 and three sums stand in DVE's queue ahead of its left part, and the sums came at 0.84 where GpSimd ran. Behind both waits the fc1 took 1.5 us longer at half clock, a cost that no term held. Block 0 came 6 us over its terms; the relu-first kernel brought it from 96.2 to 92.6 and e10, with its other edits, to 88.8.
- **Part 2**, the tails block, is the step that failed; it mis-sized what the shared port costs and put the cost on the wrong engine. From 412.97 to the end of the pair with the next block's fc1, 68.1 was forecast, 77.4 measured. The step said "GpSimd becomes the bound" and took DVE's holds as a toll of 1.9 on GpSimd per pair, period 7.8. Four pairs, from the fc1 at 422.08 to that at 457.45, take 8.84 each. GpSimd is busy 29.2 of these 35.4, DVE 31.4. The toll is mostly paid by DVE, whose 128 columns go from 0.30 to 0.60 and 256 from 0.42 to 0.80, 21 us over the block, and it is DVE's lateness that relu and fc1 wait for, not the right's low part, as the second sign had it. By itself, in e1 and e2, DVE is busy 4.7 per pair and the pair takes 6.37, GpSimd 6.7 and 7.38; the two don't fit into either period together. The pairs up to there took 51.5, forecast 47.6. The last two pairs took 25.9, forecast 20.5; their first x wait is 2.86 behind DVE's late queue, and transposes, products and the first fc1 of block 2 ran at half clock, about 4 us.
- The **Trainium skill**, SBUF — State Buffer, section "Who interferes with whom", gives the first who comes the port pair for its whole instruction. The prediction weighed this against [rows 5], worked out a period of about 9 and 8 us more, and set it aside. The trace agrees with the page in this: 8-column instructions last until GpSimd's ends, and the period is 8.84. That 68.1 + 8 = 76.1 comes so near to 77.4 is in part luck, since 5.4 of the 9.3 missing lie in the last two pairs, about 4 of them the clock. The row had shown both losses, 0.17 for GpSimd and 1.2 for DVE (1.61 instead of 0.41); the prediction's period priced the first and left out the second.
- The last step, **960 instead of 963.8** because "some of these waits will overlap with one another", went the wrong way: the measured sum lies above the terms, and several waits cost clock besides.
- Adding up, measured less forecast: tails block and boundary +9.3, block 0 +6.2, last block and v tiles +1.8, the rest of MLP 2 +2.5 (1.4 of it the u products' clock), attention +1.2 (within what its end moved from run to run, 309.6 to 311.4 at hidden(0,0)), blocks 2 and 3 +0.2: 21.2, which with the 23.0 makes 44.2 of the 44.4 between the spans.
- Rivals: A and B priced the port at nothing or little, and are refuted by e1 and e2. C, the lock in the full blocks, was right in its mechanism (0.74 and 0.82 in full blocks too) and wrong in its place: pairs there have room, 10.51.

## What to carry to other kernels

Where DVE instructions with two SBUF inputs run beside GpSimd, compare the sum of the two engines' durations, not either engine, with what TensorE needs. Here the sum, 4.7 + 6.7 = 11.4 per pair, is the bound from above, 8.84 was measured, and TensorE needed 5.4. When sums on the other engines are to save TensorE columns, look for room in each stage and for banks: here the full blocks had room for the sums, but their saving went into the x transposes on a single bank, and the tails block had room for neither. (That more banks would save the full blocks is not shown; only the plain tails block had them.) Where TensorE is the bound, add to a wait like those here, 2.2 to 3.6 us, the 1.3 to 1.6 us that the matmuls behind it mostly lost.

## What was not expected of the hardware

- **DVE's tensor_scalar with one SBUF tensor as input** (its two scalars are [128, 1]) is held up as well: the normalising of 512 columns takes 546 ns with GpSimd small and 944 beside it. The statistics (673 and 674), instructions with a PSUM input (680, and 683 in the kernel before) and ScalarE's copies (404 and 401 for 256 columns) are not touched.
- **The clock behind a wait is not the same each time.** Waits of 2.93, 2.88 and 2.80 at the start (the changed kernel, e5, e6) were followed by fc1 of 4.42, 4.50 and 4.58, and the shorter one of 2.65 in e9 by one of 4.32. A wait of 2.71 was followed by one of 2.99 in e3 and of 4.45 in e8. Block 0 took 96.2 and, in e3, 93.2 for that reason; a difference of this size in one profile says nothing without the granted clock beside it.
- **A busy figure can be a wait.** DVE's 63.8 busy us in the tails block held 21 of waiting for GpSimd that no wait column shows.
